# Reordered planning, scatters, weight splitting and gating in a fused attention, mixture-of-experts and MLP kernel

## What is computed

```python
# 1. attention: batch 2, 8 heads, 576 positions, head_dim 64, causal window of 128, a distance bias per head
scores = where(mask, scale * q @ k.T + bias, -1e9); attn = softmax(scores); x = (attn @ v)     # 1152 tokens x 512
# 2. mixture of experts: 8 experts, 512 -> 1024 -> 512, top 1, capacity 288 tokens each
expert = argmax(x @ w_gate); gate = softmax(x @ w_gate)[expert]
disp[e, n] = x of the n-th token of expert e      # tokens beyond the capacity are dropped
y = relu(disp @ w1[e]) @ w2[e];  out[token] = gate * y[expert, place]
# 3. MLP: 512 -> 2048 -> 512
h = out @ w_in;  result = (h * sigmoid(h)) @ w_out
```

## Time and profile before

| | us |
|---|---|
| median of three runs | 448.08 |
| the profiled execution | 448.26 |
| its span (first to last instruction) | 446.2 |
| PE busy | 433.1 (97%) |
| PEld (weight loads) busy | 395.8 (89%) |
| POOL busy | 233.2 (52%) |
| ACT busy | 223.7 (50%) |
| DVE busy | 219.6 (49%) |
| PE's share of the chain that ended last | 80% |
| POOL's share of that chain | 10% |

### The profile page before, as it was taken

One profiled execution on the slowest core, in us unless ns is written; L12 is line 12 of the kernel. 1 busy time (PEld: TensorE's weight loads), 2 busy tenths in 40 slices (PEclk: granted clock), 3 DMA queues, 4 the chain that ended last, 5 costly groups with the idle time before them and its releaser, 6 DMA issues.

```text
span 446.2 us, 8319 instructions
## 1 busy us (share of the span) xinstructions
PE 433.1 (97%) x2928; PEld 395.8 (89%) x2928; DVE 219.6 (49%) x728; ACT 223.7 (50%) x547; POOL 233.2 (52%) x173
## 2 busy tenths in 40 slices
PE   7999899999999999999999999999999999999994
PEld 6687677789999999999999998999998999999893
DVE  4587687778576485675763323232323232323230
ACT  4878678756766575676676543232222222322221
POOL 5004778588998988989999986402000002000002
PEclk9999999999999999999999999999999999999998
DMA  9998991139988768878868200001000001000002
GB/s 179 268 284 224 282 291 26 48 114 354 349 306 284 237 206 290 301 258 270 307 239 290 82 1 0 2 0 71 1 0 0 0 0 71 0 0 0 0 0 76
DMA packets 54247, 63.70 MB, mean 143 GB/s; under 512 B 32064, under 2 KB 32064, under 8 KB 54208
## 3 DMA queue, kind: packets, MB, share of 16 engines
q1 hardware_dynamic: 51392, 58.23, 42.2%
q0 software_dynamic: 1776, 4.73, 3.0%
q10 hardware_dynamic: 1040, 0.26, 0.3%
HBM read 53.76 MB, written 9.44 MB: 142 GB/s over the span
## 4 chain that ended last, share of the span: by engine, by line
PE 80%; POOL 10%; ACT 5%; DVE 2%; issue 2%; POOLq 0%; DVEq 0%
PE bank L1316 15%; PE bank L1317 15%; PE bank L1318 15%; PE bank L1338 12%; POOL w_lo L498 9%; PE bank L1337 5%; ACT prob L627 3%; PE bank L1146 3%; PE bank L1335 2%; PE bank L1163 2%; PE bank L1197 2%; PE bank L1185 2%; PE bank L1130 1%; PE bank L1336 1%; ACT kT L616 1%
## 5 line engine op out<-in xcount | busy, mean ns | idle before, releaser
L498 POOL TENSOR_TENSOR w_lo<-w_raw,w_hi 128x1024 fp32r<-128x1024 f32 x73 | 174.4, 2421 | 15.4 <-DVE w_lo L1068 6.5
L598 POOL DMA_INDIRECT out_dram<-out_stage,permcol x9 | 8.7, 972 | 149.6 <-ACT out_stage L768 148.5
L657 ACT ACTIVATE w_hi<-w_raw 128x1024 fp32r<-128x1024 f32 x76 | 80.0, 1053 | 0.0
L1099 DVE TENSOR_TENSOR bank<-bank,sigmoid 128x384 f32<-128x384 f32 x48 | 27.2, 567 | 102.8 <-ACT sigmoid L751 100.3
L751 ACT ACTIVATE sigmoid<-bank 128x384 f32<-128x384 f32 x48 | 23.6, 492 | 98.5 <-PE bank L1318 91.6
L1028 DVE TENSOR_REDUCE bank<-bank 128x192 f32<-128x384 f32 (+5 forms) x96 | 49.2, 514 | 41.3 <-PE bank L1338 40.8
L1316 PE MATMUL bank<-x_hi,w_hi 128*128 x192 | 65.0, 338 | 0.5 <-POOL w_lo L498 0.5
L1318 PE MATMUL bank<-x_hi,w_lo 128*128 x192 | 64.6, 336 | 0.0
L1317 PE MATMUL bank<-x_lo,w_hi 128*128 x192 | 64.5, 336 | 0.0
L1338 PE MATMUL bank<-hidden,w_hi 128*128 128x384 f32 (+5 forms) x224 | 62.4, 351 | 0.0
L1338 PE MATMUL bank<-xT,w_hi 128*128 128x384 f32 (+5 forms) x192 | 56.7, 351 | 0.0
(11 more groups left out here) (154 smaller groups left out, 779.3 us busy)
## 6 DMA issues: line engine op xcount, KB each, us to landing
w_raw<-in_moe_w_dram SPq DMA_DIRECT2D x64, 512.0 KB, 5.9
dispatch_dram<-zeros SPq DMA_DIRECT2D x4, 1152.0 KB, 8.0
w_raw<-in_moe_w_in_dram SPq DMA_DIRECT2D x8, 512.0 KB, 4.3
w_raw<-in_moe_w_out_dram SPq DMA_DIRECT2D x8, 512.0 KB, 6.9
dispatched<-dispatch_dram SPq DMA_DIRECT2D x8, 384.0 KB, 7.9
q_raw<-in_q_dram SPq DMA_DIRECT2D x8, 256.0 KB, 6.5
v_raw<-in_v_dram SPq DMA_DIRECT2D x8, 256.0 KB, 7.7
k_raw<-in_k_dram SPq DMA_DIRECT2D x7, 256.0 KB, 8.3
```

The source lines that it names most:

```text
L498: nc.gpsimd.tensor_tensor(wlo[s][:, sl], raw[s][:, sl], whi[s][:, sl], ALU.subtract).then_inc(pool_lo, 1)
L657: nc.scalar.activation(whi[s][:, sl], raw[s][:, sl], ACT.Copy).then_inc(whi_ready, 1)
L1099: nc.vector.tensor_tensor(bank[f % 4][:, 0:TB], bank[f % 4][:, 0:TB], sig[:, f % 2, :], ALU.mult).then_inc(gf_ready, 1)
```

## The change

Five things are changed.

- The plan: `above` and its products go to SBUF; the chain up to `excess` reduces only the kept counts; the first output columns of the experts are worked out right after `excess` and both rows of `plan` are written in one instruction, so `plan_ready` has two values only. `output_places` loses what has moved.
- SP: two pieces of the second expert's w1 are loaded before it waits for the scatters, not one; the third part of the first expert's tokens is loaded ahead of `load_dispatched`. PE's turn of expert 0 also waits for `third_in`.
- POOL: `select_first` of tile 8 comes before the scatters, which stand together behind the wait for the last slot numbers.
- Splitting: of expert 6 (`E - 2`) POOL makes six pieces and DVE two, in one instruction of 2048 columns. POOL waits for DVE's piece ahead of all pieces of every expert.
- MLP: ACT runs `sigmoid(f)` and then `g_high(f - 1)`, DVE `g_full(f)` and then `g_low(f - 1)`.

```diff
         def pooled_by(e, n):
-            return POOLED * e + n + (1 if e > 0 else 0)
+            return sum(map(pooled, range(e))) + n
+
+        def pooled(e):
+            return SPLITS if e == 0 else POOLED - 1 if e == E - 2 else POOLED
...
             sp.wait_ge(xd_in, 16)
-            load_w1(expert[1], 2, range(1))
+            load_w1(expert[1], 2, range(2))
             sp.wait_ge(scattered, 16 * NTOK)
+            load_third(0)
             sp.wait_ge(step_done, KC)
             load_dispatched(expert[1])
-            load_third(0)
-            load_w1(expert[1], 2, range(1, PIECES))
+            load_w1(expert[1], 2, range(2, PIECES))
...
-            pool.wait_ge(xd_in, 16)
-            scatter(LAST)
             pool.wait_ge(seen_ready, NTOK)
             select_first(LAST + 1)
-            scatter(LAST + 1)
+            pool.wait_ge(xd_in, 16)
             pool.wait_ge(last_slots, NTOK - LAST)
-            scatter(LAST + 2)
+            for t in range(LAST, NTOK):
+                scatter(t)
...
                 for p in pieces:
-                    if e >= 2 and p == (1 if e == E - 1 else 0):
-                        pool.wait_ge(dve_lo, e - 1)
                     low_here(w_slot + p // PIECES, p % PIECES, split_by(e, p + 1))
-            lows(1, 2, range(POOLED))
+            lows(1, 2, range(pooled(1)))
             for e in range(2, E):
-                lows(e, 2 * (e % 2), range(POOLED))
+                pool.wait_ge(dve_lo, e - 1)
+                lows(e, 2 * (e % 2), range(pooled(e)))
+            pool.wait_ge(dve_lo, E - 1)
             lows(E, 0, range(2 * PIECES))
...
                 for f in range(F2C):                       # ACT
                     sigmoid(tb, f)
+                    if f >= 1:
+                        g_high(tb, f - 1)
                     if first and f < 2 * PIECES:
                         weight_high(2 + f // PIECES, f % PIECES, 16 * (E // 2 + 1))
-                    g_high(tb, f)
+                g_high(tb, F2C - 1)
...
-            link(nc.vector.tensor_tensor(ranked[:, 0:2], at_rank[:] ..., vals[:, 0:2] ..., ALU.mult))
-            link(nc.vector.reduce_sum(by_rank[:, 0:2], ranked[:, 0:2], axis=AX.X))
+            link(nc.vector.tensor_tensor(ranked[:, 0], at_rank[:], kept8 ..., ALU.mult))
+            link(nc.vector.reduce_sum(by_rank[:, 0, :], ranked[:, 0], axis=AX.X))
             link(nc.vector.tensor_tensor(over8[:], by_rank[:, 0, :], width8[:], ALU.subtract))
             link(nc.vector.reduce_max(over[:], over8[:], axis=AX.X))
             nc.vector.tensor_scalar_max(excess[:], over[:], 0.0).then_inc(plan_ready, 1)
-            nc.vector.tensor_copy(plan[:, 1, :], by_rank[:, 1, :]).then_inc(plan_ready, 1)
+            link(nc.vector.tensor_tensor(kept_above[:], above[:], kept8 ..., ALU.mult))
+            link(nc.vector.reduce_sum(off8, kept_above[:], axis=AX.X))
+            link(nc.vector.tensor_tensor(ranked[:, 1:3], at_rank[:] ..., vals[:, 1:3] ..., ALU.mult))
+            link(nc.vector.reduce_sum(by_rank[:, 1:3], ranked[:, 1:3], axis=AX.X))
+            nc.vector.tensor_copy(plan[:], by_rank[:, 1:3, :]).then_inc(plan_ready, 1)
...
                     if e >= 1 and (kind, c) == ("up", 1):
-                        s, sl = 2 * (e % 2) + 1, slice((PIECES - 1) * PIECE, PIECES * PIECE)
+                        s, sl = 2 * (e % 2) + 1, slice((pooled(e) - PIECES) * PIECE, PIECES * PIECE)
...
                     for f in range(F2C):                   # DVE
                         g_full(tb, f)
-                        g_low(tb, f)
+                        if f >= 1:
+                            g_low(tb, f - 1)
+                    g_low(tb, F2C - 1)
...
                         if c == 0:                         # PE, turn
                             pe.wait_ge(xd_in, 16 * e + 32)
-                            if e > 0:
-                                pe.wait_ge(third_in, 16)
+                            pe.wait_ge(third_in, 16)
```

More of the change, by code:

```diff
@@ L161, in build @@
     first8, o = at("first_bias", [P, E], F32, o)
+    above, o = at("above", [P, E, E], F32, o)
     kept_above, o = at("kept_above", [P, E, E], F32, o)
@@ L484, in _ @@
             nc.gpsimd.iota(tokid[:].rearrange("p (b i) -> p b i", b=B), [[S, B], [P, NT]], base=0, channel_multiplier=1)
-            nc.gpsimd.iota(vals[:, 1, :], [[1, E]], base=0, channel_multiplier=0, allow_small_or_imprecise_dtypes=True)
+            nc.gpsimd.iota(vals[:, 2, :], [[1, E]], base=0, channel_multiplier=0, allow_small_or_imprecise_dtypes=True)
             nc.gpsimd.iota(slot_no[:], [[1, FIRST]], base=0, channel_multiplier=0, allow_small_or_imprecise_dtypes=True)
@@ L720, in steps @@
                         if e == 0:
-                            act.wait_ge(plan_ready, 3)
+                            act.wait_ge(plan_ready, 2)
                         off = offset_of(act, e)
@@ L985, in _ @@
             dve.wait_ge(count_done, 1)
-            kept8, expert_no = vals[:, 0, :], vals[:, 1, :]
-            above = bank[COUNTS][:, P:P + E * E].rearrange("p (i j) -> p i j", i=E)
+            kept8, off8 = vals[:, 0, :], vals[:, 1, :]
             over_e = [P, E, E]
@@ L1001, in _ @@
             nc.vector.tensor_scalar_max(excess[:], over[:], 0.0).then_inc(plan_ready, 1)
-            nc.vector.tensor_copy(plan[:, 1, :], by_rank[:, 1, :]).then_inc(plan_ready, 1)
+            link(nc.vector.tensor_tensor(kept_above[:], above[:], kept8.unsqueeze(1).broadcast_to(over_e), ALU.mult))
+            link(nc.vector.reduce_sum(off8, kept_above[:], axis=AX.X))
+            link(nc.vector.tensor_tensor(ranked[:, 1:3], at_rank[:].unsqueeze(1).broadcast_to([P, 2, E, E]),
+                                         vals[:, 1:3].unsqueeze(2).broadcast_to([P, 2, E, E]), ALU.mult))
+            link(nc.vector.reduce_sum(by_rank[:, 1:3], ranked[:, 1:3], axis=AX.X))
+            nc.vector.tensor_copy(plan[:], by_rank[:, 1:3, :]).then_inc(plan_ready, 1)
             def output_places():
-                off_e, off, droprank, base_, off_r = (bank[COUNTS][:, 16 * n:16 * n + w] for n, w in
-                                                      ((1, E), (2, NTOK), (3, NTOK), (4, NTOK), (5, E)))
-                link(nc.vector.tensor_tensor(kept_above[:], above, kept8.unsqueeze(1).broadcast_to(over_e), ALU.mult))
+                off_e, off, droprank, base_ = (bank[COUNTS][:, 16 * n:16 * n + w] for n, w in
+                                               ((1, E), (2, NTOK), (3, NTOK), (4, NTOK)))
+                nc.vector.reduce_sum(droprank, over_c[:], axis=AX.X)
                 link(nc.vector.reduce_sum(off_e, kept_above[:], axis=AX.X))
-                link(nc.vector.tensor_tensor(ranked[:, 2], off_e.unsqueeze(1).broadcast_to(over_e), at_rank[:], ALU.mult))
-                link(nc.vector.reduce_sum(off_r, ranked[:, 2], axis=AX.X))
-                nc.vector.tensor_copy(plan[:, 0, :], off_r).then_inc(plan_ready, 1)
-                nc.vector.reduce_sum(droprank, over_c[:], axis=AX.X)
                 link(nc.vector.tensor_tensor(oo[:], off_e.unsqueeze(1).broadcast_to([P, NTOK, E]), onehot[:], ALU.mult))
@@ L1371, in steps @@
                         if c == 0:
-                            if e == 0:
-                                pe.wait_ge(pool_lo, SPLITS)
-                            else:
-                                pe.wait_ge(pool_lo, pooled_by(e, POOLED))
+                            pe.wait_ge(pool_lo, pooled_by(e, pooled(e)))
+                            if e > 0:
                                 pe.wait_ge(dve_lo, e)
```

11 lines of the change are left out of this document (5 added, 6 removed).

## The result

The changed kernel is slower, and slower than I forecast. Its median is 451.77 us (451.03 to 453.56, 6 runs) against 448.23 (447.14 to 451.41, 6 runs) of the kernel before beside it: ratio 1.0082 (95% interval 1.0057 to 1.0105), or +3.5 us where I had +2.1. The same kernel run again later, on another chip, gave 453.0 (451.03 to 454.69, 11 runs) against 448.72, ratio 1.0083 (1.0051 to 1.0115).

What follows compares the result with a forecast made beforehand. PE's matmuls were taken to bound the kernel, busy in three quarters of the span, so any new PE wait is paid in full. 0.40 (seam, start included) + 1.74 (block ends) = +2.1 us, median 450.2 us; range 448.3 to 451.2.

Steps and rivals of the forecast that it cites:

- The sign: Whole kernel: slower than before, chance 0.67; same 0.28.
- the five terms: The five places the change touches, taken in order of time; together +2.1 us.
- SP's order: SP's loads before PE's turn of expert 0: tokens land at 107.4, needed at 107.92; cost 0, bound +0.5 us.
- rival 3: More waits than counted: tokens +0.5, MLP block starts +0.3, 451.0 us; or a scatter holds a plan product, 451.3; chance 0.12.
- Selection and scatters: POOL before the first expert: selection gains up to 0.24 us, lost again in the plan's chain; last scatter 0.46 later.
- The plan's chain: DVE's instructions behind `excess` delay `x_low` and so the first expert's matmul: +0.25 us, bounds 0 and +0.5.
- The seam: Between experts and MLP: POOL waits for DVE's long piece; MLP starts 0.40 us later, including 0.25 from the start.
- The block ends: End of each MLP block: PE waits for chunk 14's `g_low`, 0.58 us per block, +1.74 us for three.
- 1 (no stall at the ends): MLP block ends don't stall PE: then +0.4 us, 448.5, no change; chance 0.18.
- 2 (relief of POOL): POOL's fewer pieces remove PE's 0.5 us wait before the MLP, start gains 0.13: 447.5 us at best; chance 0.10.

Runs made afterwards that it cites:

- the second trace: The changed kernel, unchanged, profiled once more; that execution took 452.13 us.
- experiment 2: MLP's order undone in the changed kernel: 450.36 us, ratio 1.0038; MLP's order alone added to the kernel before: 453.36 us, ratio 1.0052.

## Why the prediction was wrong

The sign and four of the five terms held; the total missed by more than my range, by one term.

- **SP's order** is the step that failed. I put the tokens' landing "at 107.4, half a us either way", took 0 and bounded it by +0.5. They landed at 109.9 and PE stood 1.92 us (1.73 in the second trace, 0.90 with the MLP's order undone). The mechanism was my rival 3's; its price was up to four times what I gave it. Already my own terms don't give 107.4: the 5.0 us of before and 704 KB more at 300 to 400 KB/us make 6.8 to 7.3 us of flight, so 108.0 to 108.5 from an issue at 101.2, behind the 107.92 at which PE needs them. I had put 6.2 us without a reason. Measured, the flight took 8.1 us (7.8 and 7.0 in the other two traces), and the issue was at 101.85 (101.64 without the 0.21 us by which this trace's attention stage is late) instead of 101.2, of which the scatters' order has some 0.3.
- **A consequence that I had nowhere**: after the longest stalls (1.92 and 2.66 us) the granted clock fell to half level, worth 1.63 us in the profiled execution; after 1.73, 1.14 and 0.90 it did not. The stall alone doesn't decide it: in the attention stage of the trace with SP's order undone it fell after waits of 0.79 and 1.22 us, 9 us apart. How many of the timed runs have it is open; the two traces are of executions of 454.15 us (with it) and 452.13 (without), and the medians lie at 451.77 and 453.0.
- **Selection and scatters**: the earlier selection gains nothing, as reckoned. The last scatter was to start at 97.25; it started at 97.96 by the time of the trace of before, mostly for the 0.85 us ahead of the first.
- **The plan's chain**: +0.25 forecast, from `values` to the first product 3.87 us against 3.59, +0.24 at the first product after the trace's own 0.21. The chain of DVE rows that I worked out stands as forecast, five instructions behind `excess` ahead of `x_low`:

```profile
97.06 0.15 DVE L1006 TENSOR_SCALAR excess<-over 128x1 int32<-128x1 f32 x1
...
97.96 0.28 DVE L1011 TENSOR_REDUCE by_rank<-ranked_parts 128x16 f32<-128x128 f32 x1
98.28 0.17 DVE L1012 CAST plan<-by_rank 128x16 int32<-128x16 f32 x1
98.36 1.14 DVE L1039 TENSOR_TENSOR xT<-bank,xT 128x192 fp32r<-128x192 f32 x4
```

- **The seam**: DVE's long piece took 2.28 us, the very number; POOL resumed when it ended; PE's wait there is 0.7, and the step costs 0.16 (0.15 forecast). What I did not see is its use: in part of the runs of before, up to 24 of 81 by the count above, a race is lost that costs 3.45 us, and this ends it. Alone it came with +0.38, of which 0.25 are the meeting at expert 1.
- **The block ends**: 1.62 to 1.68 us for three (1.74 forecast), shown from both sides, undone and alone.
- **Rivals**: 1 (no stall at the ends) is excluded by experiment 2; 2 (relief of POOL) is right only in that the seam's edit alone is not slower, and for a reason that I had not given.

## What to carry to other kernels

Where a load has a deadline on a saturated engine, its cover must be reckoned with both ends moved: when it is issued now, and how many bytes stand ahead of it on its queue at that moment; and the flight itself varies (7.0 to 8.1 us for one and the same start), so that 0.5 us of cover against a guess of "half a us either way" is no cover. A wait that is put ahead of several issues can hold back their preparation too. When runs of one kernel fall into two groups, look for an instruction whose duration differs between a trace of each: a wait that seems to cost something may pay by ending a race. And one group can have two causes; the granted clock told them apart here.

## What was unexpected in the hardware

- At the boundary of two of POOL's pieces a waiting DVE instruction with two SBUF inputs got in or didn't: 2.36 or 4.68 us for the same piece, in one and the same program. Of five traces of kernels without POOL's wait two lost the race, of the kernel before one of two. What decides it stays open; earlier or later starts of the experts (97.81 and 98.38 in the lost ones; 97.87, 98.32 and 98.41 in the won ones) don't sort them.
- After PE's stalls of 1.92 and 2.66 us the granted clock was at half for about 3.4 us: 1.63 and 1.60 us more (6.10 - 2.66 - 0.16 - 1.68), nearly as much again as the first stall.
- 0.85 us lie between the release of POOL's wait and the start of the indirect DMA behind it (in two traces of the changed kernel); between scatters in a row it is 0.30.
